# Round 0 of eight experts: w2 loaded behind the gather, one routing digit moved, x turned through four banks, the last scatters awaited on SyncE

## The reference, cut to what matters

```python
logits = x @ w_gate
flat = logits.flatten()
order = np.argsort(-flat)
...
for idx in order:
    tok, e = (int(idx) // E, int(idx) % E)
    if assigned[tok] >= 0 or counts[e] >= cap:
        continue
    assigned[tok] = e
    counts[e] += 1
...
for e in range(E):
    mask = assigned == e
    h = np.maximum(x[mask] @ w1[e], 0.0)
    out[mask] = h @ w2[e]
```

## Time and profile before

| | us |
|---|---|
| median of three runs | 928.96 |
| lowest and highest run | 927.03, 929.26 |
| the profiled execution | 927.07 |
| its span, first to last instruction | 925.4 |
| TensorE busy | 834.3 (90%) |
| VectorE busy | 608.5 (66%) |
| ScalarE busy | 351.6 (38%) |
| GpSimd busy | 315.0 (34%) |

### The profile page before, as it was taken

How to read it: one execution, slowest core, us unless ns; L and a number is a source line. 1 busy time by engine, 2 the same in 40 slices (tenths; PEclk the granted TensorE clock), 3 DMA queues, 4 the chain that set the end, 5 groups by cost and what they waited for, 6 DMA issues and landing times. The chain is left out here.

```text
span 925.4 us, 21404 instructions
## 1 busy us (share of the span) xinstructions
PE 834.3 (90%) x7720; PEld 757.0 (82%) x7720; DVE 608.5 (66%) x1613; ACT 351.6 (38%) x856; POOL 315.0 (34%) x325
## 2 busy tenths in 40 slices
PE   4776999999999999999999999825999999999984
PEld 3656888888889888888898999724989999999984
DVE  5886886777778767876555555466766766766520
ACT  3453333443344333433323232203445355355451
POOL 5442220221122202211000000006676786786781
PEclk9756999998999999999999999955999999999998
DMA  7873132132221320311101000005614614615600
GB/s 184 257 203 116 40 90 75 27 80 81 62 76 38 88 75 20 80 51 36 46 2 45 0 23 1 24 2 206 206 64 174 228 64 174 229 64 172 230 29 26
DMA packets 97183, 85.40 MB, mean 92 GB/s; under 512 B 64625, under 2 KB 68721, under 8 KB 97137
## 3 DMA queue, kind: packets, MB, share of 16 engines
q1 hardware_dynamic: 94064, 75.34, 26.6%
q0 software_dynamic: 3072, 9.44, 3.2%
HBM read 70.60 MB, written 14.16 MB: 92 GB/s over the span
## 5 line engine op out<-in xcount | busy, mean ns | idle before, releaser
L451 PE MATMUL PS<-xs,W 128*128 128x256 f32 x1728 | 235.6, 289 | 0.2 <-issue 0.2
L451 PEld LDWEIGHTS PS<-xs,W 128*128 128x128 f32 x1728 | 225.2, 195 | 12.0 <-issue 3.9
L451 PE MATMUL PS<-W,g 128*128 128x512 f32 x864 | 223.1, 397 | 0.0
L451 PEld LDWEIGHTS PS<-W,g 128*128 128x128 f32 x864 | 153.7, 188 | 28.3 <-issue 1.0
L541 ACT ACTIVATE a_sb<-PS,one 128x256 f32<-128x256 f32 x144 | 68.2, 474 | 252.1 <-PE PS L451 252.1
L564 DVE TENSOR_SCALAR scratch<-a_sb 128x256 f32<-128x256 f32 x144 | 52.6, 365 | 95.1 <-ACT a_sb L541 95.1
L372 POOL TENSOR_TENSOR P<-P,top 128x640 f32<-128x640 f32 x16 | 21.1, 1316 | 254.3 <-DVE top L332 254.3
L1252 POOL TENSOR_TENSOR w1s<-w1r,w1s 128x512 fp32r<-128x512 f32 x64 | 80.4, 1284 | 29.3 <-ACT w1s L1163 29.1
L1092 PE MATMUL PS<-exs,w1s 128*128 128x288 f32 x256 | 83.1, 325 | 4.9 <-DVE ehs L1217 4.9
L1268 POOL TENSOR_TENSOR w2s<-w2r,w2s 128x512 fp32r<-128x512 f32 x64 | 80.9, 1283 | 17.6 <-ACT w2s L1187 17.4
L1092 PE MATMUL PS<-ehs,w2s 128*128 128x288 f32 x256 | 80.7, 315 | 1.1 <-POOL w2s L1268 1.1
(11 more groups left out here) (166 smaller groups left out, 1426.0 us busy)
## 6 DMA issues: line engine op xcount, KB each, us to landing
w1r<-in_moe_w SPq DMA_DIRECT2D x16, 1024.0 KB, 6.0
w2r<-in_moe_w SPq DMA_DIRECT2D x8, 2048.0 KB, 9.2
qn<-in_q SPq DMA_DIRECT2D x32, 144.0 KB, 3.8
kn<-in_k SPq DMA_DIRECT2D x32, 144.0 KB, 3.6
vd<-in_v SPq DMA_DIRECT2D x16, 288.0 KB
xt<-xT SPq DMA_DIRECT2D x16, 288.0 KB, 2.2
y<-scratch SPq DMA_DIRECT2D x18, 256.0 KB, 2.0
vw<-in_v SPq DMA_DIRECT2D x68, 64.0 KB, 2.4
```

What stands on the lines that cost most here:

```text
L451: r = pe.matmul(psum, wsel(w[i]), xsel(x[j]), start=first and t == 0, stop=last and t == 2)
```

## The change

In round 0, and in round 0 alone, four things change.

- SyncE waits for the round's gather before it issues w2. For that its round 0 is written out ahead of the loop. In all rounds w2 comes in two halves with a semaphore each.
- Of routing 1 only two digits are done ahead of round 0 (EARLY_DIGITS = 2). Digit 2 stands in round 0 at steps 1 and 2, and the digits 3 to 6 shift: counts at 6, 11, 16, 21 and sums at 7, 12, 17, 22. The choice of the expert follows the last sum, as before. VectorE's round 0 is written out for that.
- x is turned through four banks, so no slice waits until an earlier one has been split.
- VectorE begins the first routing ahead of its wait for GpSimd's memsets.

At the end SyncE, and no longer GpSimd, waits for the last scatters.

```diff
-        w2_loaded = sem("w2_loaded")
+        w2_loaded = [sem(f"w2_loaded{i}") for i in range(2)]
...
         H, YB, X = bank[0:2], bank[2:4], bank[4:6]
+        FIRST_X = bank[2:6]
...
+        COUNT_FIRST = [0, 0, 1, 6, 11, 16, 21]
+        SUM_FIRST = [0, 0, 2, 7, 12, 17, 22]
...
+        def digits_at(s, r, steps, first_steps, first, following, second):
+
+            for i in range(DIG):
+                if first and i >= EARLY_DIGITS and s == first_steps[i]:
+                    yield r + 1, i
+                if s == steps[i] and (second if i < SPLIT else following and not first):
+                    yield r + 2 if i < SPLIT else r + 1, i
...
-        def pe_turn_x(pe, r, kk):
+        def pe_turn_x(pe, r, kk, X=X):
 
             pe.wait_ge(gathered, 16 * GT * r + 16 * GT)
-            pe.wait_ge(exs_lo, KC * r + kk + 1)
+            if len(X) == 2:
+                pe.wait_ge(exs_lo, KC * r + kk + 1)
...
-                act.wait_ge(w2_loaded, 16 * r + 16)
+                act.wait_ge(w2_loaded[f * 2 // EFC], 16 * r + 16)
...
-                with sp.Fori(0, E) as r:
+                def load_weights(r, first=False):
...
                     sp.wait_ge(w2_lo, EFC * r + EFC)
-                    sp.dma_start(w2r[:, :, :], w2_v[ds(e, 1), :, :, :].rearrange("a p f m -> (a p) f m")).then_inc(w2_loaded, 16)
+                    if first:
+                        sp.wait_ge(gathered, 16 * GT)
+                    for i in range(2):
+                        c = slice(i * EFC // 2, (i + 1) * EFC // 2)
+                        sp.dma_start(w2r[:, c, :], w2_v[ds(e, 1), :, c, :].rearrange("a p f m -> (a p) f m")).then_inc(w2_loaded[i], 16)
+
+                load_weights(0, first=True)
+                with sp.Fori(1, E) as r:
+                    load_weights(r)
+                sp.wait_ge(scattered, 16 * GT * E)
...
                 scatter(pool, E - 1)
-                pool.wait_ge(scattered, 16 * GT * E)
...
-                dve.wait_ge(init, 6)
-                for m, digits in ((0, DIG), (1, SPLIT)):
-                    dve_keys(dve, m)
+                for m, digits in ((0, DIG), (1, EARLY_DIGITS)):
+                    dve_best(dve, m)
+                    if m == 0:
+                        dve.wait_ge(init, 6)
+                    dve_hot(dve, m)
+                    dve_key_digits(dve, m)
...
-                with dve.Fori(0, E - 2) as r:
+                dve_round(dve, 0, first=True)
+                with dve.Fori(1, E - 2) as r:
                     dve_round(dve, r)
...
+EARLY_DIGITS = 2
```

More of the change, by code:

```diff
@@ L947, in dve_over @@
                               thr[:, i, :].unsqueeze(1).to_broadcast([128, TILES, RADIX]), ALU.is_ge).then_inc(over_ready, 1)
[L949 to L952, removed]
         def dve_best(dve, m):
@@ L1084, in experts @@
         TURN_LAST = 3
-        def assigned(r, i):
-            return r + 2 if i < SPLIT else r + 1
+        def digits_at(s, r, steps, first_steps, first, following, second):
[4 more added lines that the diff above has]
+                    yield r + 2 if i < SPLIT else r + 1, i
         def parts(pe, psum, wh, wl, xh, xl, first, last):
@@ L1094, in parts @@
             return pe.matmul(psum, wl, xh, start=False, stop=last)
-        def pe_turn_x(pe, r, kk):
+        def pe_turn_x(pe, r, kk, X=X):
             pe.wait_ge(gathered, 16 * GT * r + 16 * GT)
-            pe.wait_ge(exs_lo, KC * r + kk + 1)
+            if len(X) == 2:
+                pe.wait_ge(exs_lo, KC * r + kk + 1)
             for c in range(GT):
-                x = pe.transpose(X[kk % 2][:, c * GP:(c + 1) * GP], xg[:, c, kk * 128:(kk + 1) * 128], ident[0:GP, 0:GP])
+                x = pe.transpose(X[kk % len(X)][:, c * GP:(c + 1) * GP], xg[:, c, kk * 128:(kk + 1) * 128], ident[0:GP, 0:GP])
             x.then_inc(x_turned, 1)
@@ L1141, in pe_round @@
                         x.then_inc(ey_ready, 1)
[L1142 to L1147, removed]
+                for m, i in digits_at(s, r, COUNT, COUNT_FIRST, first, following, second):
+                    pe_count(pe, m, i)
+                for m, i in digits_at(s, r, SUM, SUM_FIRST, first, following, second):
+                    pe_sum(pe, m, i)
                 if not first and s == TURN_LAST:
@@ L1163, in act_w1, with act_x @@
             act.activation(w1s[0][:, :, c], w1r[:, :, c], ACT.Copy).then_inc(w1_hi, 1)
-        def act_x(act, r, kk):
+        def act_x(act, r, kk, X=X):
             act.wait_ge(x_turned, KC * r + kk + 1)
-            act.activation(xs[0][:, kk, :], X[kk % 2][:, 0:CAP], ACT.Copy).then_inc(exs_hi, 1)
+            act.activation(xs[0][:, kk, :], X[kk % len(X)][:, 0:CAP], ACT.Copy).then_inc(exs_hi, 1)
         def act_yt(act, r, d):
@@ L1200, in act_round, with dve_x, dve_round @@
                         act_x(act, r + 1, 3)
-        def dve_x(dve, r, kk):
+        def dve_x(dve, r, kk, X=X):
             dve.wait_ge(exs_hi, KC * r + kk + 1)
-            dve.tensor_tensor(xs[1][:, kk, :], X[kk % 2][:, 0:CAP], xs[0][:, kk, :].bitcast(F32), ALU.subtract).then_inc(exs_lo, 1)
-        def dve_round(dve, r, following=True, second=True):
+            dve.tensor_tensor(xs[1][:, kk, :], X[kk % len(X)][:, 0:CAP], xs[0][:, kk, :].bitcast(F32), ALU.subtract).then_inc(exs_lo, 1)
+        def dve_round(dve, r, first=False, following=True, second=True):
+            last_sum = SUM_FIRST[DIG - 1] if first else SUM[DIG - 1]
             for s in range(STEPS1 + STEPS2):
[L1208 to L1213, removed]
+                for m, i in digits_at(s, r, COUNT, COUNT_FIRST, first, following, second):
+                    dve_full(dve, m, i)
+                for m, i in digits_at(s, r, SUM, SUM_FIRST, first, following, second):
+                    dve_digit(dve, m, i)
                 if s < STEPS1 and s % KC == KC - 1:
@@ L1219, in dve_round @@
                 if following:
-                    if s == SUM[DIG - 1]:
+                    if s == last_sum:
                         dve_choose(dve, r + 1)
-                    if s == SUM[DIG - 1] + 3:
+                    if s == last_sum + 3:
                         dve_ahead(dve, r + 1)
@@ L1327, in _ @@
                 for kk in range(KC):
-                    act_x(act, 0, kk)
+                    act_x(act, 0, kk, FIRST_X)
                 act_round(act, 0, first=True)
@@ L1349, in _ @@
                 for kk in range(KC):
-                    dve_x(dve, 0, kk)
-                with dve.Fori(0, E - 2) as r:
+                    dve_x(dve, 0, kk, FIRST_X)
+                dve_round(dve, 0, first=True)
+                with dve.Fori(1, E - 2) as r:
                     dve_round(dve, r)
@@ L1366, in _ @@
                 for kk in range(KC):
-                    pe_turn_x(pe, 0, kk)
+                    pe_turn_x(pe, 0, kk, FIRST_X)
                 pe_round(pe, 0, first=True)
```

## The result

The changed kernel took 925.85 us in the median of 22 runs (921.81 to 929.73), the kernel before 929.48 beside it (926.12 to 935.41). The ratio is 0.9949 with a 95% interval of 0.9931 to 0.9967: 0.5% faster, 4.7 us by the ratio. The profiled execution took 921.81 us, its span is 920.1, where before had 927.07 and 925.4.

What follows compares the result with a forecast made beforehand. Taken as bounding: the wait chain from 600 to 640.7 us into round 0 and 4 us after the last scatter. 3.6 + 0.85 - 0.65 - 0.7 + 1.8 = 4.9 us takes the median 928.96 to 924.1; range 921.8 to 927.6.

Steps and rivals of the forecast that it cites:

- the rival in which the drain keeps its end: Kernel's end: GpSimd's drain ends no earlier although SyncE takes the wait; gain 3.1 us, time 925.9, chance 0.22.
- routing starts earlier: Start of round 0's routing: VectorE's first operations run ahead of the memset wait, 0.77 us won, bounds 0.7 to 0.8.
- first transpose earlier, this included: Round 0's turning of x: with w2 held back the gather lands at 634.4, 3.6 us earlier, the 0.77 included.
- four banks: Round 0, first transpose to first expert matmul: twelve transposes run without a break, 0.85 us won.
- digit between the matmuls: Block 0 of round 0: the moved digit's small matmuls and sum cost TensorE 0.65 us.
- wait at step 28: Round 0, step 28: TensorE waits for VectorE's split behind the later digit sum; 0.7 us lost, bounds 0.3 to 0.9.
- clock (what is left): TensorE's clock rise around block 0: taken as 0, between some 0.4 us lost and up to 1.2 won.
- rounds behind step 28: After step 28 and in rounds 1 to 7: nothing moves, so round 0's gain or loss arrives at the end whole.
- the end: After the last scatter: GpSimd drains earlier because SyncE takes the wait; 1.8 us won if the drain is fixed.
- second rival: Round 0's gather: w2 only thins it out; gain 2.1 to 2.6 us, 926.4 to 926.9; chance 0.15, both rivals together included.
- w2 in halves: Round 0's w2 load: first half there by 640.4, just in time for ScalarE, GpSimd's w1 covering tenths; priced at nothing.
- Slower, by instruction loads: VectorE around round 1: instruction loads stuck behind weights stop it 4.5 us each; 931 us and more, chance 0.08.

Runs made afterwards that it cites:

- hold alone: Kernel before, with only SyncE's wait for round 0's gather ahead of w2 (one piece) added: 926.66 us in a single run; retimed on another chip 941.63 us, 0.9980 of before.
- the wait on GpSimd: Changed kernel with the last wait for the scatters back on GpSimd instead of SyncE: 942.85 us in a single run, on a chip where the kernel before takes 944.82.

## Why the prediction was right, step by step

It said 924.1 (921.8 to 927.6) and most likely faster; it is 925.85. The time alone doesn't decide for the forecast, since the rival in which the drain keeps its end gave 925.9; the tail does, 7.10 us before and 5.14 after. Each term, from the stages of the two profiles:

| term | predicted | measured |
|---|---|---|
| routing starts earlier | 0.77 | 0.70 |
| first transpose earlier, this included | 3.6 | 3.40 |
| four banks | 0.85 | 0.84 |
| digit between the matmuls | -0.65 | -0.92 |
| wait at step 28 | -0.7 | -0.54 |
| clock (what is left) | 0 | 0.0 |
| rounds behind step 28 | 0 | 1.46 |
| the end | 1.8 | 1.96 |
| sum | 4.9 | 6.2 |

- **The gather.** I chose 3.0 us to landing, by the quickest gather, against today's 5.8; TensorE went on 3.11 behind the last issue. That the three go as one, which spoke for the second rival, was wrong: without w2 the first packet comes at 631.65, ahead of the last issue at 632.46. Taking the row with no packet for a queue that is held, and not thinned out, was the step that decided between the forecast and its second rival.
- **The digit.** The next matmul came 0.55 us behind the count's start and 0.09 behind the sum's. That is 0.64, at the lower clock, as forecast. What I had left out is that each of these two matmuls then takes 0.38 us to the next instead of 0.24 (639.59 to 639.97, 640.55 to 640.93), another 0.28.
- **Step 28.** The mechanism was right, the size somewhat too large. From the matmul ahead of step 28 to its first it is 0.70 us now (653.42 to 654.12) and 0.16 before (655.82 to 655.98), so 0.54 lost, of which the timeline shows 0.41 as idle. I took the choice's length from the trace of before less a little. The member mask took 0.23 us in round 0 of after, as no split of GpSimd stood beside it, and 0.39 before (L1002 there), where it ended 0.03 us behind one.
- **The clock.** I had named a loss of 0.4, with a gain of 1.2 as the other end, and took 0. The rise came 5.5 us behind the first transpose again (641.1 against 635.57, before 643.5 against 638.01), the case of the loss. But what runs at the lower level for longer is the digit, whose row has that price already: eleven of the expert's matmuls start ahead of the rise now, as before. With the digit and step 28 counted from start to start nothing is left for the clock.
- **w2 in halves.** The halves were priced at nothing, and ScalarE waits for neither. A whole w2 cost 0.6 to 0.7 at step 28 in its run: the cover that I named, GpSimd's w1, didn't hold, since ScalarE's next split of a block is queued behind the copy.
- **Rounds 1 to 7.** Here a term was missing: I took it that nothing moves behind round 0. From start to start 1.21 of the 1.46 us lie at the transposes for round 1, which waited for their gather (1.03 of it idle). That wait is in the profile of before alone, in none of the experiments', with w2 of round 0 held or not. That gather stands behind round 1's own w2, as round 0's did: by the rows below 76 packets of the weights still move later than 1 us after the last gather's issue (668.21 to 674.21 us, before), and none after the change (666.25 to 672.25). In the four profiles with w2 in one piece it is 19 to 76, in the ten with halves 0 to 26. So the halves may be what shortens it, but the counts overlap, and hold alone, with w2 in one piece, waits only 0.05 us: it isn't shown. 0.16 lie at a count in the second half of round 0, where TensorE waits for `over`. It stands idle for 0.28 us there before and 0.27 with hold alone, the two kernels in which VectorE's round 0 is in the loop, and for 0.11 to 0.12 in the four others whose rounds take 34.7 us; why, I didn't test. Some 0.1, the rest, has no owner.
- **The end.** The drain follows GpSimd's last instruction by 4.0 us, and the wait for the landing no longer stands ahead of it. The rival that the drain waits for the transfer falls with the wait on GpSimd: its drain begins after the landing and takes 3.98 all the same.
- **Slower, by instruction loads.** VectorE has no such pause: from 664 to 705 us its idle stretches are at most 1.24 us, and each ends with TensorE, ScalarE or itself. The rival didn't show.

The transfers behind round 1's last gather, by queue (packets, MB, share), before:

```profile
q0 software_dynamic: 163, 0.48, 24.5%
q1 hardware_dynamic: 76, 0.15, 8.2%
```

and after:

```profile
q0 software_dynamic: 129, 0.37, 20.7%
```

The profiles differ by more than the medians: 4.26 + 1.96 = 6.2 us in the stages, less 0.95 of the dense part, is the 5.26 between the profiled executions, while the medians differ by 3.6. The profiled execution of the changed kernel is the fastest of its 22 runs, that of before lies 2.4 us under its median. Whether the wait for round 1's gather is in the other runs of before no profile shows; if it isn't, it accounts for 1.03 of the difference. The rest lies within the runs' spread of some 8 us.

So the mechanism held stage by stage, and the closeness of the number is in part luck: the forecast terms alone gave 4.7 us in the profiles against 4.9, with errors of 0.2 and 0.3 to the one side (transposes, digit) and of 0.2 and 0.2 to the other (step 28, the end), and the missing 1.46 came on top in a pair of profiles that differ by more than the medians do.

## What to carry to other kernels

A transfer that someone waits for goes ahead of a large one that nobody needs yet, even on another queue; look for the stretch in which its queue has no packet. Then ask who is free to use it: here the hold was worth 0.36 us at step 28 by itself, and 1.64 once a digit had been moved out of the way. A wait for a landing ahead of a fixed drain belongs on an engine that has nothing to drain.

## What I hadn't expected of the hardware

- GpSimd's first gather packet came 1.83 to 1.86 us behind the first issue with no load beside it, and 4.38 to 4.52 with 2 MB of weights queued on SyncE's queue.
- GpSimd's drain at the block's end takes 4.0 us behind its last instruction: its own length is 3.98 behind a wait, and it ends 3.99 behind the end of a scatter's issue as behind that of a memset of 0.11 us.
- An operation of VectorE on 18 numbers a row took up to 1.56 us beside GpSimd, and 0.22 in a form that reads PSUM.
- The kernel before took 931 us on one chip and 943 to 945 on three others. In the profiles taken there TensorE waits up to 1.7 us for VectorE's `full`, which follows its count. Each of the three was timed later than the first, so the chip and the hour aren't told apart, and the cause stays open.
